# Zero stores behind the row stores, and the second expert's weights behind the gate column, in an attention and two-mixture kernel

## The reference, cut to what matters

```
# 1. attention: 8 heads, each token a softmax-weighted sum of itself and 6 tokens before
w = softmax(weight_gen)                       # [2, 3584, 8, 7]
x = einsum('bshk,bskhg->bshg', w, x_unfolded)
# 2. noisy mixture of 8 experts, two per token
noisy = x @ w_gate + log1p(exp(x @ w_noise)) * noise
top2  = argpartition(-noisy, 2)[:, :2]; g = softmax of the two
out[t] = sum over the two experts e of  g * (relu(x[t] @ w1[e]) @ w2[e])
# 3. mixture of 8 other experts, one per token, by cosine similarity to embeddings
```

## Time and profile before

| | |
|---|---|
| time, median of 3 runs | 1172.62 us (1170.9 to 1174.1) |
| the profiled execution | 1180.06 us, of which 1178.2 us are the span from the first to the last instruction |
| TensorE busy | 1064.8 us, 90% of the span |
| VectorE, ScalarE, GpSimd busy | 729.1, 525.6 and 593.7 us |
| moved by DMA | 98.76 MB, 84 GB/s on the mean |
| mean granted TensorE clock | 0.961 of full speed |

### The profile page before, as it was taken

The page is one execution under the profiler, slowest core; times in us unless marked ns, Lnnn a source line. Parts: engine busy times, 40 slices in busy tenths (PEclk is TensorE's granted clock), DMA queues, the critical chain, the costliest instruction groups (busy, mean ns, idle before and its releaser), DMA issues.

```text
span 1178.2 us, 27653 instructions
## 1 busy us (share of the span) xinstructions
PE 1064.8 (90%) x7845; PEld 999.5 (85%) x7845; DVE 729.1 (62%) x1473; ACT 525.6 (45%) x1391; POOL 593.7 (50%) x723
## 2 busy tenths in 40 slices
PE   1889347999999999999999999988399999999997
PEld 0566237999999999999999999954199999999997
DVE  8999584556565655656556565556656565567663
ACT  2122253445454544545445454425255454456553
POOL 6888003555555655565555655520034444444443
PEclk9999768999999999999999999989599999999999
DMA  9766793225352352423435334361431331133511
GB/s 332 178 160 166 150 3 87 44 40 103 41 104 39 44 103 40 102 42 47 98 42 100 44 51 92 40 164 39 8 92 41 101 86 56 43 87 111 154 45 32
DMA packets 105846, 98.76 MB, mean 84 GB/s; under 512 B 30899, under 2 KB 96746, under 8 KB 105532
## 3 DMA queue, kind: packets, MB, share of 16 engines
q1 hardware_dynamic: 76412, 62.08, 23.7%
q0 software_dynamic: 29376, 35.97, 18.0%
HBM read 63.82 MB, written 34.98 MB: 84 GB/s over the span
## 4 chain that ended last, share of the span: by engine, by line
PE 82%; DVE 7%; DMA 6%; POOL 3%; issue 2%; ACT 1%; DVEq 0%; POOLq 0%; SPq 0%; ACTq 0%
PE banks L714 23%; PE banks L716 11%; PE banks L700 9%; PE banks L702 7%; PE banks L706 7%; PE banks L701 7%; PE banks L705 7%; DMA token_rows<-gate 3%; PE banks L638 3%; DVE prods L988 3%; POOL prods L475 2%; PE banks L684 2%; PE banks L685 2%; PE banks L619 2%; DMA x_slots<-token_rows,gather_idx 1%
## 5 line engine op out<-in xcount | busy, mean ns | idle before, releaser
L1165 DVE SCALAR_TENSOR_TENSOR h_lo<-banks,h_hi 128x256 fp32r<-128x256 f32 x736 | 312.1, 424 | 336.4 <-ACT h_hi L891 297.5
L891 ACT ACTIVATE h_hi<-banks 128x256 fp32r<-128x256 f32 x736 | 282.7, 384 | 419.6 <-PE banks L706 386.9
L714 PE MATMUL banks<-w_hl,h_hi 128*128 128x384 f32 x1472 | 465.8, 353 | 0.0
L716 PE MATMUL banks<-w_hl,h_lo 128*128 128x192 f32 x1472 | 367.5, 250 | 0.0
L716 PEld LDWEIGHTS banks<-w_hl,h_lo 128*128 128x128 f32 x1472 | 279.4, 190 | 0.0
L714 PEld LDWEIGHTS banks<-w_hl,h_hi 128*128 128x128 f32 x1472 | 276.7, 188 | 0.2
L487 POOL DMA_INDIRECT x_slots<-token_rows,gather_idx x188 | 188.9, 1005 | 112.2 <-POOL gather_idx L480 81.7
L506 POOL DMA_INDIRECT token_rows<-y_slots,store_idx x120 | 193.6, 1614 | 84.7 <-issue 58.0
L700 PE MATMUL banks<-x_hi_a,w_hi 128*128 (+1 forms) x736 | 226.7, 308 | 0.0
L706 PE MATMUL banks<-x_hl_b,w_lo 128*128 (+1 forms) x736 | 207.4, 282 | 0.0
L701 PE MATMUL banks<-x_hi_a,w_lo 128*128 (+1 forms) x736 | 207.3, 282 | 0.0
(11 more groups left out here) (177 smaller groups left out, 1156.1 us busy)
## 6 DMA issues: line engine op xcount, KB each, us to landing
raw<-in_moe_w SPq DMA_DIRECT2D x17, 768.0 KB
token_rows<-stage SPq DMA_DIRECT2D x28, 384.0 KB, 5.1
raw<-in_moe_w SPq DMA_DIRECT2D x17, 512.0 KB
raw<-in_moe_w SPq DMA_DIRECT2D x34, 256.0 KB
token_rows<-zeros SPq DMA_DIRECT2D x14, 386.0 KB, 6.9
x_halo<-in_x SPq DMA_DIRECT2D x2, 2688.0 KB, 15.3
rows<-token_rows SPq DMA_DIRECT2D x14, 384.0 KB, 7.3
x_slots<-token_rows,gather_idx POOLq DMA_INDIRECT x188
```

The lines of the kernel that those rows point to most:

```text
L714: mm(y[:, i, 0:2 * D], h_hi[:, c % HBUFS, t], w2_hl[u][:, c, :, :], start=c == 0, stop=False)
L716: ins = mm(y[:, i, 0:D], h_lo[:, c % HBUFS, t], w2_hl[u][:, c, 0, :], start=False, stop=c == FC - 1)
L891: sc.activation(h_hi[:, c % HBUFS, :], banks[:, c % HBANKS, 0:BLOCK], ACT.Relu).then_inc(h_hi_ready[m], 1)
L1165: v.scalar_tensor_tensor(h_lo[:, c % HBUFS, :], banks[:, c % HBANKS, 0:BLOCK], 0.0, h_hi[:, c % HBUFS, :].bitcast(F32), ALU.max, ALU.subtr ...
```

## The change

In SP's program, the zero stores are taken out of the loop over the groups: the loop now has the row stores alone, and behind it SP waits for `zeros_ready` and issues all 14 zero stores, and then that of the padding. And the loads of the second expert's weights, with their wait for `weights_ready`, go from ahead of the wait for the gates to behind the two stores of the gate column. Nothing else differs; all other engines' programs are as before.

```diff
                 sp.wait_ge(rows_ready, g + 1)
                 for k in range(CHOICES[0]):
                     sp.dma_start(tile_rows(token_rows[0], k * T + g * GROUP, GROUP)[:, :, 0:D], stage[g % 2][:]).then_inc(rows_stored[g % 2], 16)
-                if g == 0:
-                    sp.wait_ge(zeros_ready, 1)
+            sp.wait_ge(zeros_ready, 1)
+            for g in range(NG):
                 zero_rows(g * GROUP * P, GROUP)
             zero_rows(N, DUMP_ROWS // P)
...
+            sp.wait_ge(gates_ready[0], 1)
+            store_gates(0)
             sp.wait_ge(weights_ready, 1)
             load_expert(w1, w2, 1)
-            sp.wait_ge(gates_ready[0], 1)
-            store_gates(0)
             with sp.Fori(2, E) as e:
```

## The result

| | median | range | runs |
|---|---|---|---|
| before | 1173.01 us | 1170.9 to 1174.1 | 6 |
| after | 1181.01 us | 1180.7 to 1182.2 | 6 |

The ratio of after to before is 1.0072, with a 95% interval of 1.0059 to 1.0085: +8.0 us against the medians. The sign is as forecast. The size is not: 20.0 us were forecast, two and a half times as much, and the time is close to that of rival 1 (1182.0), whose chance was 0.27.

The account below looks back on a forecast made before the run. The gate column's store was taken to end the stretch before the first gather; zeros 18.2 + column 0 + gather 1.8 gave +20.0 us on a median of 1172.62: 1192.6 us, range 1176.5 to 1200.

Parts of the forecast that it names:

- rival 1: Zeros behind the last row store move at a burst's 178 GB/s; column delayed 7.6 us, with gather 9.4: 1182.0 us; chance 0.27.
- What bounds: Before the first gather, GpSimd waits for the gate column, so any delay of it adds to the time one for one.
- Zeros out of the loop: In the attention loop, fewer SP issues and less traffic gain under 1 us, taken as 0.
- Zeros behind the last row store: In SP's queue ahead of the gate column, 5.73 MB at 134 GB/s outlast 24.6 us of cover: +18.2 us.
- The Trainium skill's bandwidth: For the moved zeros, 341 GB/s would end them at about 145, hidden before the gate column.
- The column itself: The gate column's 14336 packets stay some 22 us of transfer: 0 taken, up to +3 us.
- The weights behind the column: Second expert's loads run beside GpSimd's first gather and slow it: +1.8 us, between 0 and +3.9; ScalarE does not wait.
- SP held by a full queue: While SP issues the zeros, a full queue might hold it, but the column would begin no sooner or later.

Follow-up runs that it names:

- run 3: Kernel before with only the zeros moved behind the last row store, second expert's weights loaded early, behind group 11, then group 10: 1.0075, then 1.0056.
- run 4: The changed kernel, unedited, measured again beside its parts: 1187.09 us, 1.0093 against the kernel before.
- run 7: Changed kernel with the first seven groups' zeros kept in the loop (half): 1179.42 us; with four more zero stores behind the fifteen (more): 1195.33 us.
- run 5: Kernel before with the second choice's gates not stored behind the routing, zeros stored there during attention group 0 instead: 1196.95 us, with more blocks.
- run 2: Kernel before with only the second expert's weight loads moved behind the gate column, zeros still in the loop: 1179.67 us, 1.0030.
- run 9: Changed kernel with the second expert's weight loads put between the zeros and the gate column: 1188.37 us, 1.0104 against the kernel before.
- run 6: Changed kernel with the zero stores issued by GpSimd on its own queue after the last row sum: 1185.74 us, 1.0081 against the kernel before.
- run 8: Kernel before with the second choice's gate column issued by ScalarE on its own queue, the first staying with SP: 1175.9 us, 0.9992.
- run 1: The kernel before, unedited, measured again for a second profile: 1176.3 us, 0.9997.

## Why the prediction was wrong in size and right in kind

**What bounds: right.** The gate column ended the stretch in the profile, and what delayed it was added to the time: runs 3, 4 and 7 give the slope, run 5 the floor. That the median execution of before was 7 us shorter than the profiled one was seen and not asked about. It was partly a long column: a column time of 25.5 us, against 22.5 to 24.1 in the other profiles with an idle queue. The end of the attention stage varies between profiles as well, with TensorE's granted clock in 60 to 90 us. Where it is 1.00 throughout, the last row sum starts at 121.2 to 121.4 (runs 2, 7 half, and 9); where it falls to 0.94 on the mean, at 122.6 to 123.9 (ten profiles, both first ones among them). VectorE waits 1.2 us there, which the profiles at 1.00 don't show. The kernels do the same in this stretch but for the zero stores, and either level occurs with and without them:

```profile
60.00:90.00 30.00, 26.14 (x123) 17.35 (x122) 29.39 (x18) 7.02 (x17) 26.60 (x18) 1.00 0.55 145
```

```profile
60.00:90.00 30.00, 26.16 (x120) 17.71 (x118) 28.50 (x17) 7.27 (x18) 25.48 (x17) 0.94 0.33 106
```

(The levels are 1.00, 2.4 GHz, and 0.50, 1.2 GHz; 0.94 is a mean with some 3.6 us at the lower one.) In the first profile of before the clock is lower from about 75.5 to 79 us, right after TensorE had waited 2.3 us for GpSimd's sums; but the profiles at 1.00 have the same wait of 2.3 us. Why it falls in some executions and not in others is open.

**Zeros out of the loop: right.** No gain; the steps of the attention stage stay at 6.82 us.

**Zeros behind the last row store: the failed step.** The mechanism and the place held, and the 24.6 us of cover nearly; the rate did not. I took 134 GB/s, by the row of 128.5 to 133, because it was "the only one taken 10 us into such traffic", and read its fall as that of a long burst. The changed kernel moved zeros for 26 us at 191 GB/s, the runs at 176 to 186. The row was low for another reason: the weight loads stood right behind those zeros in the queue. Without them the same zeros ran at 217 GB/s in their first 2 us and some 187 over nearly all of them (run 2), and loads put behind the long burst brought 186 down to 135 (run 9). The change took just these loads away from there, so the row described a state that the change ended. With 5.73 MB at 186 GB/s, 30.8 us, the same sum gives 128.5 + 30.8 = 159.3, a delay of 6.2 us, and 1180.6 with the gather, 0.4 us from the measured value. That it hits the value so closely is partly luck. In the profile of after the row stores, with no zeros among them, ran at 300 GB/s and more and were moved by about 127, not 128.5, and the zeros were over by 157, not 159.3: the start of the sum was 1.5 us late as well. By the column times the delay is 5.5 to 6.7 us in the later sessions (29.1 and 30.3 against 23.6), but in the first session's profile of after it is only 2.5 (26.1 against 23.6), and there some 3.7 of the 8.0 us are in neither the column nor the gather. Since the profiles agree within 3.3 us behind the first gather, that rest probably lies before it, in an ordinary execution of before in the first session, of which there is no profile. Single profiles scatter by 3 us in the column and by 2.7 in the attention stage, and the rest isn't settled.

**The Trainium skill's bandwidth** ("DMA: Bandwidth & Descriptors", section Bandwidth) lay too high for these stores, as the prediction's rows said: 341 GB/s, measured there for loads, against 176 to 191 here. The Trainium skill's section Queues, rings and completion order, on the same page, has an engine take turns between the queues that it has work for. Runs 6 and 8 don't show that: with zeros in GpSimd's queue, SP's queue moved nothing for 4 us after its issue, and ScalarE's nothing for 5 us beside SP's column. With a gather beside a load, where it was weighed for the price of the gather, the measured 4.5 to 5.5 us are about the double of 2.65 that it allows.

**The column itself: 0 taken, right within its scatter.** In an idle queue its packets took some 22 us in the first profile of before and 19 to 20.5 in runs 1, 2, 7 (half) and 8; behind the zeros some 19 in after (156 to 175) and 21 to 23 in runs 3, 4 and 6. In run 4 the packets fall to 243 in the one us from 167 and are back at 1052 in the next, between the two stores of the column; after and run 3 have the same dip, the columns in an idle queue don't. Whether it makes the difference was not tried.

**The weights behind the column: right in kind, low in size.** The gather was put at +1.8 (the middle of 0 to 3.9 is 1.9) and measured +1.84 in after, but 2.6 in run 2 and 2.9 in run 4; ScalarE does not wait at line 863. The prediction had itself found that the load covers the whole gather, which speaks for the upper half. The part alone costs 3.1 to 3.5 us.

**SP held by a full queue: seen as harmless, and it was,** though the issues took 24.86 us. Had the zeros lasted longer, SP would have come late to the gates, with the queue still full: run 7's more shows it, with the column issued from 160.4 and still no gap.

**Range and rivals.** Rival 1 (burst rate, 178) was the true one, in mechanism and in size. Its argument for, 173 GB/s on the mean in every period of the loop, was the reading taken over most microseconds and most bytes; I preferred the last 4.5 us of the burst to it.

## What to carry to other kernels

Take the rate of a transfer from a stretch whose queue has the same neighbours before and behind as it will have after the change; here loads queued behind stores cost the stores a quarter of their rate. Work moved into an idle stretch of the queue is free only up to a threshold, cover times rate, and behind it every byte counts; compute the threshold with the sustained rate. And where a small late transfer ends a stretch, look first at whether its data could be ready earlier: three instructions of VectorE moved up were worth 6.6 us, where no reordering of the transfers tried here gained anything.

## What the runs showed of the hardware that was not expected

- Stores of zeros into DRAM held 191 GB/s for 26 us in after and 176 to 186 over 10 us and more in runs 3, 7 and 9; they fell to 135 GB/s as soon as loads out of DRAM were issued behind them (run 9), at a DMA share that stayed at 1.14 to 1.17.
- That rate was nearly the same with 6864 packets as with 1354, and a column in another queue got nothing through until those stores were all but over (run 6). The second half of a column in ScalarE's queue waited 5 us in the same way for the first half in SP's (run 8).
- A store of 14336 values of 4 bytes took 19 to 23 us of transfer, some 3 GB/s, and no less when split over two queues (run 8).
- SP was held in issuing 15 stores for 24.86 us, where 15 undisturbed issues would take 11.5; the queue takes only some stores ahead of the transfers.
- In 14 profiles TensorE's granted clock in 60 to 90 us was 1.00, 0.94 or once 0.89, and the attention stage's last row sum began at 121.2 to 121.4, 122.6 to 123.9 and 126.4 us; the last had more in the queue at the beginning (run 5).
- The same kernel had medians of 1173.0 in one session and 1175.6 to 1176.7 in the others, and the same change cost 8.0 us in the first and 10.8 in a later one.
